# Preparing the first MLP stage inside the attention steps

## The reference

```python
# attention, per batch and head
q_d, k_d, v_d = means of q, k, v over groups of 4 positions
out_up    = repeat(softmax(q_d @ k_d.T / 8) @ v_d, 4)
out_local = softmax(q @ k.T / 8 where |i - j| < 4) @ v
x = (out_up + out_local) as [2304 tokens, 512]
# first MLP
h = ((x @ w1) * (x @ w2)) @ w3          # w1, w2: 512 x 1024, w3: 1024 x 1024
x = h @ w_out                           # 1024 x 512
# second MLP
h = x @ w_in                            # 512 x 2048
out = (h / (1 + exp(-h))) @ w_out2      # 2048 x 512
```

## Time and profile before

| | us |
|---|---|
| median of 3 runs | 854.91 |
| the runs | 854.04, 859.28, 854.91 |
| profiled execution | 858.21 |
| its span | 856.2 |
| TensorE busy in it | 824.0 |

### The profile page before, as it was taken

How to read it: one execution, slowest core, us unless ns; L and a number is a source line. 1 busy time by engine, 2 the same in 40 slices (tenths; PEclk the granted TensorE clock), 3 DMA queues, 4 the chain that set the end, 5 groups by cost and what they waited for, 6 DMA issues and landing times.

```text
span 856.2 us, 14971 instructions
## 1 busy us (share of the span) xinstructions
PE 824.0 (96%) x5584; PEld 736.0 (86%) x5584; DVE 605.9 (71%) x974; ACT 336.7 (39%) x605; POOL 293.1 (34%) x355
## 2 busy tenths in 40 slices
PE   4899999879999999999999999999999999999998
PEld 4778888668999999998999988898898899889897
DVE  3567787777667677677767966777876777866654
ACT  3655565443335222443335423235333235333232
POOL 5776666684231422332221332130331220321100
PEclk9899999989999999999999999999999999999999
DMA  7756676302111110111112221221421221511202
GB/s 182 203 134 160 159 170 162 85 25 75 31 44 50 50 50 29 46 51 50 40 35 85 83 80 50 74 74 50 150 72 50 82 67 50 172 50 50 74 1 74
DMA packets 128724, 68.88 MB, mean 80 GB/s; under 512 B 63393, under 2 KB 117153, under 8 KB 128673
## 3 DMA queue, kind: packets, MB, share of 16 engines
q1 hardware_dynamic: 128672, 68.18, 28.2%
HBM read 63.44 MB, written 4.72 MB: 80 GB/s over the span
## 4 chain that ended last, share of the span: by engine, by line
PE 81%; DVE 10%; POOL 3%; issue 3%; ACT 1%; DMA 0%; DVEq 0%; SPq 0%; POOLq 0%; ACTq 0%
PE ps L1034 36%; PE ps L1092 22%; PE ps L1063 11%; PE ps L1190 4%; PE ps L1107 2%; PE ps L1172 2%; DVE mu L874 1%; DVE wa L742 1%; PE ps L1117 1%; PE ps L1156 1%; DVE a L880 1%; DVE g L886 1%; PE ps L1128 1%; PE ps L1198 1%; POOL r L411 1%
## 5 line engine op out<-in xcount | busy, mean ns | idle before, releaser
L1034 PE MATMUL ps<-xb,wa 128*128 128x384 f32 x2016 | 408.0, 339 | 6.1 <-POOL wa L492 2.3
L1034 PEld LDWEIGHTS ps<-xb,wa 128*128 128x128 f32 x2016 | 356.2, 189 | 30.3 <-DVE mu L874 3.8
L424 POOL TENSOR_TENSOR rw<-rw 128x256 f32<-128x256 f32 x48 | 44.6, 930 | 440.9 <-DMA rw<-in_moe_w_in 210.5
L874 DVE TENSOR_TENSOR mu<-ps,mu 128x384 f32<-128x384 f32 x132 | 73.2, 554 | 129.9 <-PE ps L1034 129.3
L1063 PE MATMUL ps<-g,r 128*128 128x512 f32 (+1 forms) x576 | 125.6, 339 | 1.6 <-DVE g L886 1.0
L1092 PE MATMUL ps<-w2h_even,g 128*128 128x512 f32 x432 | 113.8, 394 | 1.5 <-DVE osb L919 1.5
L638 ACT ACTIVATE a<-a 128x384 f32<-128x384 f32 x72 | 37.9, 526 | 191.7 <-DVE a L874 191.7
L1092 PE MATMUL ps<-w2h_odd,g 128*128 128x512 f32 x432 | 112.5, 393 | 0.0
L1063 PEld LDWEIGHTS ps<-g,r 128*128 128x128 f32 x576 | 97.1, 188 | 12.3 <-issue 2.7
L742 DVE TENSOR_TENSOR wa<-rw,wa 128x1024 fp32r<-128x1024 f32 x94 | 104.2, 1109 | 1.9 <-ACT wa L501 1.7
L1092 PEld LDWEIGHTS ps<-w2h_even,g 128*128 128x128 f32 x432 | 79.6, 188 | 14.1 <-DVE osb L919 2.4
(11 more groups left out here) (87 smaller groups left out, 883.5 us busy)
## 6 DMA issues: line engine op xcount, KB each, us to landing
rw<-in_moe_w SPq DMA_DIRECT2D x48, 256.0 KB, 3.1
rw<-in_moe_w_in SPq DMA_DIRECT2D x48, 256.0 KB, 3.2
w2r<-in_moe_w_out SPq DMA_DIRECT2D x48, 256.0 KB, 2.9
qn<-in_q SPq DMA_DIRECT2D x32, 144.0 KB, 3.1
kn<-in_k SPq DMA_DIRECT2D x32, 144.0 KB, 3.3
vw<-in_v SPq DMA_DIRECT2D x32, 144.0 KB, 3.0
out<-osb SPq DMA_DIRECT2D x18, 256.0 KB, 2.2
wn<-in_moe_w SPq DMA_DIRECT2D x16, 256.0 KB, 3.3
```

Source lines behind the costliest of these rows:

```text
L424: nc.gpsimd.tensor_tensor(blocks[:, 4, :], blocks[:, 0, :], blocks[:, 1, :], ALU.add).then_inc(s1_ready, 1)
L874: nc.vector.tensor_tensor(o, half_bank(k, i), term, ALU.add).then_inc(sum_ready, 1)
L1034: e = nc.tensor.matmul(ps[:, (k + i) % 2, 0:TH], wa[:, k % 2, l, A_SLOT[i], a * P:(a + 1) * P], xb[:, i, r, a, :], start=(i in (0, 1, 4) a ...
```

## The change

- The loop is cut to steps 3 to 10 (`AHEAD` is 10), and steps 11 to 14 are written out behind it with the same instructions. There VectorE makes one token sum of tile 0 at the end of each step, and GpSimd two of a set's four sums: set 0's in steps 11 and 12, set 1's in 13 and 14. Both weight loads move ahead of the inputs of pairs 12 and 14 on SyncE's queue.
- In step 15 the transposes of the last half of w3 stand before the weighted part, ScalarE makes the first two high token parts at its beginning and the high part of w3's last half at its end.
- In step 16 the last product of w3 and w_out goes to bank `pS`, and so waits for the exponentials that read that bank and no longer for the split of bank `pW`. The transposes of probabilities come between the two halves' products. Set 0's low weights are made by VectorE.
- GpSimd's sums of set 2 wait for a VectorE addition of set 0, as the later stages' did already.

```diff
-            with eng.Fori(1, PAIRS // 2 - 1) as i:
+            with eng.Fori(1, AHEAD // 2) as i:
+                step(i, 1, True, True, True, (i - 1, 1), (i, 0))
+                step(i, 2, True, True, True, (i, 0), (i, 1))
+            for i in range(AHEAD // 2, PAIRS // 2 - 1):
...
-            load_weights(0)
-            load_weights(1)
+            with sp.Fori(2, AHEAD // 2 + 1) as i:
+                load_pairs(i)
+            for n in range(2):
+                load_weights(n)
+                load_pairs(AHEAD // 2 + 1 + n)
...
             def step(i, c, turn, score, weigh, mul, flip):
-                if not turn:
-                    sums(0)
...
+                if isinstance(s, int) and AHEAD < s <= AHEAD + 4:
+                    sums((s - AHEAD - 1) // 2, (s - AHEAD - 1) % 2)
...
-            pool.wait_ge(wa_hi, 1)
-            for n in range(7):
-                e = nc.gpsimd.tensor_tensor(wa[:, 0, 1, n, :], rw[:, 0, 1 + n, :], wa[:, 0, 0, n, :].bitcast(F32),
-                                            ALU.subtract)
-            e.then_inc(wa_lo, 1)
-            for k in range(1, SETS):
-                if k % PER == 2 and k > PER:
+            for k in range(2, SETS):
+                if k % PER == 2:
                     pool.wait_ge(sum_ready, 5 * (k - 2) + 2)
-                sums(k)
+                sums(k, 0)
+                sums(k, 1)
...
+                if score and not turn:
+                    act.wait_ge(q_turned, PAIRS)
+                    tokens_high(0, 0)
+                    act.wait_ge(k_turned, PAIRS)
+                    tokens_high(0, 1)
                 if last:
-                    w3_high((MT - 1, 1), pT)
-                    tokens_high(0, 1)
-                    act.wait_ge(vt_ready, PAIRS)
-                    tokens_high(0, 2)
                     act.wait_ge(scored, 2 * PAIRS)
                     act.wait_ge(pooled, 2 * PAIRS)
-                    tokens_high(0, 3)
                     act.wait_ge(masked, PAIRS)
                     act.wait_ge(w3_turned, 2 * MT)
                     act.wait_ge(vd_ready, PAIRS)
                     weights_high(0)
+                    tokens_high(0, 2)
...
+                if last:
+                    tokens_high(0, 3)
...
                 if not turn and not score:
-                    take_w3((MT - 1, 1), pT)
-                    token_sum(0, 2)
-                    token_sum(0, 3)
                     tokens_low(0, 0)
                     tokens_low(0, 1)
+                    weights_low(0, 0)
+                    weights_low(0, 1)
                     tokens_low(0, 3)
...
-                    take_w3o(MT - 1)
+                    take_w3o(MT - 1, pS)
...
                 if not turn and score:
+                    take_w3((MT - 1, 1), pT)
+                if isinstance(s, int) and AHEAD < s <= AHEAD + 4:
                     dve.wait_ge(x_ready, 3 * 2 * HP)
-                    token_sum(0, 0)
-                    token_sum(0, 1)
+                    token_sum(0, s - AHEAD - 1)
...
-                        if h == 0:
+                        if last:
+                            pe.wait_ge(exp_d, PAIRS)
+                        elif h == 0:
                             pe.wait_ge(w3o_lo, m)
...
-                        e = nc.tensor.matmul(ps[:, pW, :], w3t[:, l, a, :], r3[:, a, r, :],
+                        e = nc.tensor.matmul(ps[:, pS if last else pW, :], w3t[:, l, a, :], r3[:, a, r, :],
...
                     for a in range(4):
                         multiply(a)
+                    turn_local()
+                    turn_down()
                     multiply(0, (MT - 1, 1))
                     multiply(1, (MT - 1, 1))
-                    turn_local()
-                    turn_down()
                     weighted_local_waits()
...
+                if score and not turn:
+                    turn_w3((MT - 1, 1), pT)
                 if weigh:
...
-                if score and not turn:
-                    turn_w3((MT - 1, 1), pT)
```

More of the change, by code:

```diff
@@ L205, in attention_then_mlps @@
         block = ctx.enter_context(nc.Block())
+        AHEAD = PAIRS - 6
         def steps(eng, step):
@@ L336, in _, with load_pairs @@
             load_windows(2, 0, False)
-            with sp.Fori(2, PAIRS // 2) as i:
+            def load_pairs(i):
                 load_q(2 * i, 0, False)
@@ L418, in _, with sums @@
             pool.wait_ge(blank, 3)
-            def sums(k):
+            def sums(k, half):
                 blocks = rw[:, k % 2, :, :]
[L423 to L433, removed]
+                if half == 0:
+                    pool.wait_ge(rw_in[k % 2], 32 * (k // 2) + 32)
+                    nc.gpsimd.tensor_tensor(blocks[:, 4, :], blocks[:, 0, :], blocks[:, 1, :], ALU.add
+                                            ).then_inc(s1_ready, 1)
+                    nc.gpsimd.tensor_tensor(blocks[:, 6, :], blocks[:, 2, :], blocks[:, 0, :], ALU.subtract
+                                            ).then_inc(s3_ready, 1)
+                else:
+                    pool.wait_ge(s1_ready, k + 1)
+                    nc.gpsimd.tensor_tensor(blocks[:, 5, :], blocks[:, 4, :], blocks[:, 2, :], ALU.subtract
+                                            ).then_inc(s2_ready, 1)
+                    pool.wait_ge(s2_ready, k + 1)
+                    nc.gpsimd.tensor_tensor(blocks[:, 7, :], blocks[:, 3, :], blocks[:, 5, :], ALU.subtract
+                                            ).then_inc(s4_ready, 1)
             def step(i, c, turn, score, weigh, mul, flip):
@@ L601, in step @@
                     copy_act(gate_a[:, 0:1], ident[0:1, 0:1])
-                    copy_act(r2_block(m, 0), ps[:, pW, :]).then_inc(w3o_hi, 1)
+                    copy_act(r2_block(m, 0), ps[:, pS if last else pW, :]).then_inc(w3o_hi, 1)
                 if score and not turn:
[L604 to L607, removed]
+                    w3_high((MT - 1, 1), pT)
                 if last:
@@ L796, in take_local, with take_w3o @@
                     ).then_inc(x_ready, 1)
-                def take_w3o(m):
+                def take_w3o(m, bank=pW):
                     dve.wait_ge(w3o_hi, m + 1)
-                    nc.vector.tensor_tensor(r2_block(m, 1), ps[:, pW, :],
+                    nc.vector.tensor_tensor(r2_block(m, 1), ps[:, bank, :],
                                             r2_block(m, 0).bitcast(F32), ALU.subtract).then_inc(w3o_lo, 1)
@@ L1181, in multiply @@
                     m, h = mul
+                    last = not turn and not score
                     if part == 0:
```

## The result

| | kernel before | changed kernel |
|---|---|---|
| median | 855.53 us (4 runs, 854.04 to 859.28) | 847.38 us (4 runs, 846.90 to 848.48) |
| profiled execution, its span | 858.21, 856.2 us | 847.36, 845.5 us |
| median of a later set | 856.56 us (14 runs) | 848.26 us (6 runs) |

The ratio is 0.990, 95% interval 0.9866 to 0.9934; in the later set 0.9895, 0.9864 to 0.9926. That is 8.2 and 8.3 us against a forecast of 8.5; the time of 847.4 lies in the range of 844.6 to 850.6. It is on the 1% line, as forecast.

A forecast was written before the change was run, and what follows sets the result against it. TensorE, busy 824.0 of 856.2 us, bounds the kernel; only its idle time or slow products can be won. Terms -4.5 - 4.3 + 0.3 = -8.5 us take the median 854.91 to 846.4, range 844.6 to 850.6.

The forecast's parts named there:

- Part A: End of TensorE's attention work (P): comes at 175.5 instead of 179.99, 4.5 us less.
- the mask: Step 15's mask on VectorE, delayed by step 14's token sum: TensorE waits 0.5 us (bounds 0 and 1.0).
- The wait that I named as late next: TensorE's last attention step: wait for step 15's down exponentials and the split of w3 half (7,0), costed at nothing.
- Part B: From the end of TensorE's attention to product 7 of set 0: 8.3 us instead of 12.56, 4.3 less.
- The contention of 0.5: VectorE's chain to product 7: 0.5 us added because GpSimd's sums of set 2 run beside its end.
- Part C: Steps 11 to 14 taking in token and weight sums: 0.3 us charged for all of it, bounds 0 and 2.
- the forecast's own signs: Right if steps 12 to 15 begin at most 0.5 later; wrong if GpSimd's shift or normalization, or q's DMA, releases pauses.
- Rival 1: Attention steps: mask, shift and q each a little late, 0.6 to 0.9 a step; time 849.4 to 850.9; chance 0.11.
- Rival 2: Entry after attention: VectorE's token and weight splits wait out one GpSimd sum each; gain 7.6, time 847.3; chance 0.06.
- Rival 3: Last attention step: exponentials or w3 split still 3 us late, clock falls; gain 4.0, time 850.9; chance 0.04.
- Rival 4: Steps 11 to 15: GpSimd becomes the bound, losing 8.4 to 11.6; slower, time 858 to 862; chance 0.04.
- Rival 5: More is won: no contention, no wait on the mask; gain 9.7 to 10.5, time 844.4 to 845.2; chance 0.05.

The follow-up runs named there:

- the second profile: The changed kernel run again with nothing altered, against the kernel before: median 848.26 us (6 runs), ratio 0.9895 (0.9864 to 0.9926).
- loop cut only: The kernel before with only steps 11 to 14 written out, same instructions and order, against the kernel before: 854.72 us, ratio 0.9988 (0.9972 to 1.0004).
- sums in steps 9 to 12: The changed kernel with token and weight sums in steps 9 to 12 instead of 11 to 14: 847.99 us, ratio 0.9904 to the kernel before.

## Why the prediction held

**The frame held**: the two preparation pauses went, and nothing in the MLP stages gave them back except 0.8 us (0.54 in set 1, where VectorE's additions were late once by 0.69, and 0.25 spread over the rest; in the second profile 0.24 and 0.10).

**Part A.** The pauses of 3.00 and 0.26 and the slow products went. With the loop cut alone, 15.20 us lie between step 15's last product group (160.76) and P (175.96); in the changed kernel 9.74, and 0.4 more is spent ahead of it for the moved transposes. So the handover itself is worth 5.0 us, the forecast's 5.0 without the mask. For the last step itself I had worked out 9.12; it measured 9.0. The wait that I named as late next did not appear.

**Part B** was 4.09 for 4.3: VectorE's chain was mis-sized by 0.2, P to product 7 being 8.47, not 8.3. The contention of 0.5 in it is real (1.49 for 0.95 at 179.05); starting set 2 later removed 0.54.

**Part C is the step that failed, twice, in opposite directions.** I charged 0.5 for step 15's mask and 0.3 for the rest. Measured to the start of step 15's last product group, from the start of step 11: loop cut only 43.49, with the transposes' 0.42 it would be 43.91; changed kernel 46.58. The sums cost 2.7 us. I took VectorE's 1.2 us of idle time as room for a token sum of at most 1.54; it was 2.24, and the mask, the minimum and the split of w3 were late with it. GpSimd's sums cost as much as VectorE's: cutting either returned 1.2. On the other side, "the unrolled steps run the same instructions" missed that the idle time in front of VectorE's addition would go with the loop, worth 1.2 us (1.0 in steps 12 and 14, 0.24 in the pause behind them). Net 1.5, where I had 0.8. By the forecast's own signs this part was wrong: step 15's first product came 38.55 us after the start of step 11 and 37.2 before, 1.3 later and not at most 0.5, and q's DMA stood as a releaser inside these steps (0.23).

**How much of it is luck.** The forecast of 8.5 was added up from step 11 on. The traces give 6.9 and 7.4 there (6.9 in the first profile, 7.4 in the second), the medians 8.2 and 8.3. The rest, some 0.8 to 1.3 us, comes from nothing that the forecast names, and no run settles where it arises. So the time fell close to the forecast partly by luck.

**The rule that I weighed and did not follow.** The Trainium skill ("SBUF — State Buffer", Who interferes with whom) says that a VectorE instruction with two SBUF inputs and a GpSimd instruction that reads SBUF exclude each other for the whole instruction, and that the first one wins. Here the trace agrees: 64 elements in 1.50 us behind a normalization and 0.21 ahead of one; the normalization in 1.79 us, not 1.15, the other way round. In one point the runs go beyond it: a VectorE instruction that waits can be passed by the next GpSimd instruction too, as in the 2.24 and the 1.50, though not always (at 179.05 it waited for one sum only). I had read "0.3 to 0.6 longer" out of the earlier trace rows as a rate; those rows were instructions that had come partly late. The page also says that a `tensor_scalar` can take part in this, in the modes in which it uses both of VectorE's ports, and the `tot` row of 0.73 for 0.17 fits that. For product 7 the rule's price (0.9 smaller) was too high: only one of the two late splits met a GpSimd instruction.

**Rivals.** Rival 1 (attention steps pay 0.6 to 0.9 a step) was half right: 2.7 over five steps, 0.5 each. Rival 2's time of 847.3 is the one measured (847.38), and its exclusion is real; but it priced it at the entry, where one split lost 0.54, while most of the loss came in steps 11 to 15, so its match is chance as well. Rival 3 did not come. Rival 4 had the engines push each other, which they did, but GpSimd did not become the bound: 2.7 us lost in place of 8.4 to 11.6, and cutting its sums returned only 1.2 of them. Rival 5 (9.7 to 10.5) did not come.

## What to carry to other kernels

Work that fills an engine's idle time is not free if it uses a path that another engine needs: look for what the other engine is doing at that instant, and price the meeting as what is left of the instruction that came first, and perhaps the next one in its queue (2.24 us for 0.95 here). Moving preparation out of the handover, together with a free bank for the last product, removed pauses of 3.00 and 2.33 us; the steps that took the sums in paid 2.7 us for it, and two steps earlier they paid about as much. A pause costs more than its length if the clock falls with it. Before charging a written-out loop at nothing, look for idle time in the loop body whose releaser is the instruction just before it on the same engine: here 0.43 us of it went with the loop, and TensorE gained 0.5 us in every second step.

## What was not expected of the hardware

- The length of a pause does not tell whether the clock falls behind it. One of 1.75 us was followed by products at full speed (12 in 3.01 us), and so was one of 2.25 (loop cut only: 1.00 in 170 to 190). Those of 2.33, 2.50, 2.77 and 3.00 us were followed by 0.83, 0.79, 0.83 and 0.83 over 10 us. But one of 1.41 (sums in steps 9 to 12) was followed by 0.83 too, where 1.43 at the same place in the changed kernel left 1.00; and 7 of the 50 executions of the kernel before in the later sets, whose profile has the pauses of 3.00 and 2.33, had a mean clock of 1.000. No run here shows on what else it depends.
- The code ahead of step 11, the same in nearly all these kernels, took up to 6.7 us more from one execution to another, by slow clock and by waits for DMAs. A single profile can't be compared with another by its span.
